# Attention, two gated layers, one core: per-lot waits before reloads, third lots behind the last store, and the last gate/value product inside the first output product

## What is computed

```python
# attention: B=4, HEADS=8, SEQ=576, HD=64; causal, window of 128 keys, ALiBi bias
scores = q @ k.T / 8 + slope[head] * -(i - j)        # only 0 <= i - j < 128
x = softmax(scores) @ v                              # -> 2304 tokens x 512
# layer 1: 512 -> 1024 -> 512
h = x @ w_in
solu = h * softmax(h)
x = (layernorm(solu) * g_ln) @ w_out
# layer 2: 512 -> 1536 -> 512
g = x @ w_gate
out = (g * sigmoid(g) * (x @ w_val)) @ w_out2
```

## Time and profile before

| | |
|---|---|
| median of 3 runs | 733.56 us (733.63, 731.66, 733.56) |
| the profiled execution | 733.14 us, of which span 731.4 us |
| granted TensorE clock, mean | 0.998 of full |
| TensorE busy | 715.9 us, 98% of the span |
| VectorE, ScalarE, GpSimd busy | 66%, 57%, 53% |
| the gate/value matmuls (L608) | 1512 matmuls, 505.6 us by their rows |
| the output matmuls (L767) | 756 matmuls, 254.6 us by their rows |

### The profile page before, as it was taken

How to read it: one execution, slowest core, us unless ns; L and a number is a source line. 1 busy time by engine, 2 the same in 40 slices (tenths; PEclk the granted TensorE clock), 3 DMA queues, 4 the chain that set the end, 5 groups by cost and what they waited for, 6 DMA issues and landing times.

```text
span 731.4 us, 13246 instructions
## 1 busy us (share of the span) xinstructions
PE 715.9 (98%) x4744; PEld 685.7 (94%) x4744; DVE 479.1 (66%) x850; ACT 415.5 (57%) x847; POOL 387.0 (53%) x398
## 2 busy tenths in 40 slices
PE   6999999999999999999999999999999999899998
PEld 5778999999999999999999999999999999899998
DVE  2887777777777777666885656555555699644551
ACT  5897777777777776474634433344443486345340
POOL 3567444445445445874938958759576918300000
PEclk9999999999999999999999999999999999999999
DMA  9723354433343323034234343324326753795722
GB/s 328 261 81 136 116 181 137 141 118 126 118 118 140 130 73 115 15 116 144 77 105 134 117 139 105 140 70 152 107 102 243 274 199 137 263 407 201 260 100 87
DMA packets 49340, 109.92 MB, mean 150 GB/s; under 512 B 3984, under 2 KB 30352, under 8 KB 49296
## 3 DMA queue, kind: packets, MB, share of 16 engines
q1 hardware_dynamic: 49296, 109.33, 43.3%
HBM read 75.11 MB, written 34.21 MB: 149 GB/s over the span
## 4 chain that ended last, share of the span: by engine, by line
PE 89%; DVE 3%; POOL 3%; DMA 2%; ACT 2%; issue 1%; SPq 0%; POOLq 0%; ACTq 0%; DVEq 0%
PE banks L608 35%; PE banks L594 14%; PE banks L567 14%; PE banks L767 14%; PE banks L553 4%; PE banks L539 2%; PE banks L580 2%; PE banks L530 2%; PE banks L531 2%; PE banks L517 2%; POOL st_sums L1498 2%; DMA lot_raw<-unit_scratch 1%; ACT xs_hi L783 1%; DMA unit_scratch<-st_sums 1%; DMA early<-in_first 1%
## 5 line engine op out<-in xcount | busy, mean ns | idle before, releaser
L608 PE MATMUL banks<-xs_hi,w_hi 128*128 128x384 f32 x504 | 168.8, 335 | 0.6 <-ACT g_sum L783 0.6
L608 PE MATMUL banks<-xs_hi,w_lo 128*128 128x384 f32 x504 | 168.4, 334 | 0.0
L608 PE MATMUL banks<-xs_lo,w_hi 128*128 128x384 f32 x504 | 168.4, 334 | 0.0
L608 PEld LDWEIGHTS banks<-xs_hi,w_hi 128*128 128x128 f32 x504 | 94.6, 188 | 1.6 <-ACT g_sum L783 1.1
L608 PEld LDWEIGHTS banks<-xs_lo,w_hi 128*128 128x128 f32 x504 | 94.6, 188 | 0.0
L608 PEld LDWEIGHTS banks<-xs_hi,w_lo 128*128 128x128 f32 x504 | 94.6, 188 | 0.0
L767 PE MATMUL banks<-lot_hi,wo_hi 128*128 128x384 f32 x252 | 85.1, 338 | 2.9 <-ACT out_a L783 2.2
L594 PE MATMUL banks<-lnt_hi,wout_hi 128*128 (+1 forms) x288 | 85.5, 297 | 0.0
L767 PE MATMUL banks<-lot_hi,wo_lo 128*128 128x384 f32 x252 | 84.8, 336 | 0.0
L767 PE MATMUL banks<-lot_lo,wo_hi 128*128 128x384 f32 x252 | 84.7, 336 | 0.0
L783 ACT ACTIVATE g_sum<-banks 128x384 f32<-128x384 f32 x84 | 41.1, 490 | 73.6 <-PE banks L608 56.6
(11 more groups left out here) (99 smaller groups left out, 1725.7 us busy)
## 6 DMA issues: line engine op xcount, KB each, us to landing
lot_raw<-unit_scratch SPq DMA_DIRECT2D x63, 384.0 KB, 4.9
qk_raw<-in_qk SPq DMA_DIRECT2D x28, 768.0 KB, 4.3
unit_scratch<-st_sums SPq DMA_DIRECT2D x18, 576.0 KB, 4.2
unit_scratch<-st_even SPq DMA_DIRECT2D x18, 384.0 KB, 2.5
unit_scratch<-st_odd SPq DMA_DIRECT2D x18, 384.0 KB, 3.2
w_raw<-in_wb SPq DMA_DIRECT2D x12, 512.0 KB, 4.5
v<-in_v SPq DMA_DIRECT2D x18, 256.0 KB, 2.6
x_scratch<-x_out SPq DMA_DIRECT2D x18, 256.0 KB, 2.6
```

Source lines behind the costliest of these rows:

```text
L608: last = mm(ps[n % 2], w_of[l][:, k * P:(k + 1) * P], x_of[r][:, k * HALF:(k + 1) * HALF], start=start and k == 0 and i == 0, stop=k == 1 ...
```

## The change

There are three edits.

1. `wait_stored` gets a lot number and waits only for the two chunk pairs of that lot, and SyncE's order is rewritten: the third lots of products 7 and 14 (lots 23 and 44) are loaded one step later than the first and second, and `store_pair(LAST - 2)` goes from step 1 to step 3, behind the loads of lots 21, 22, 24 and 25.
2. On TensorE, `product_3(LAST)` goes from behind the 18 matmuls of `out_product(0, 0)` to behind its first 9.
3. On ScalarE, at step `TILES`, the last two of six `xs_hi` copies of block 0 go behind `keep_p1(0)` and `keep_p7(0)`.

```diff
--- before.py
+++ after.py
@@ -283,11 +283,11 @@
                 if m >= 0:
                     eng.wait_ge(st_sent[m % 2], 48 * (m // 2 + 1))
 
-        def wait_stored(eng, j):
-
-            last = PAIRS.index(ORDER.index((C2 - 1, j)))
-            for b in range(2):
-                eng.wait_ge(st_sent[b], 48 * len(range(b, last + 1, 2)))
+        def wait_stored(eng, j, lot):
+
+            for c in (4 * lot + 1, 4 * lot + 3):
+                m = PAIRS.index(ORDER.index((c, j)))
+                eng.wait_ge(st_sent[m % 2], 48 * (m // 2 + 1))
 
         def op_ready(g):
 
@@ -441,8 +441,8 @@
                     sp.wait_ge(p3_ready, LAST + 1)
                 if g >= RING // LOTS:
                     sp.wait_ge(*op_ready(g - RING // LOTS))
-                if k % (7 * LOTS) == 0:
-                    wait_stored(sp, g // 7)
+                if g % 7 == 0:
+                    wait_stored(sp, g // 7, k % LOTS)
                 sp.dma_start(lot_raw[k % RING][:, :],
                              u_d[g // 7, OUT_OPS[g % 7][0], k % LOTS].rearrange("p h n -> p (h n)")
                              ).then_inc(lot_in[k % RING], 16)
@@ -479,11 +479,16 @@
                     sp.dma_start(out_d[rows, cols][:, :HALF], out_a[p][:, :]).then_inc(a_sent[p], 16)
 
             for g in range(OPS):
-                if g + RING // LOTS < OPS:
-                    for k in range(LOTS):
-                        load_lot(LOTS * (g + RING // LOTS) + k)
-                if g == 1:
-                    store_pair(LAST - 2)
+                ahead = g + RING // LOTS
+                if ahead < OPS:
+                    for k in range(LOTS - 1):
+                        load_lot(LOTS * ahead + k)
+                    if g == 3:
+                        store_pair(LAST - 2)
+                    if ahead % 7 == 1:
+                        load_lot(LOTS * ahead - 1)
+                    if ahead % 7:
+                        load_lot(LOTS * ahead + LOTS - 1)
                 if g == 5:
                     store_pair(LAST)
                 if g % 7 >= 4:
@@ -734,7 +739,7 @@
                     pe.wait_ge(solu_done, TILES)
                 period(n)
 
-            def out_product(g, p):
+            def out_product(g, p, chunks=range(CHUNKS2)):
 
                 j, o = g // 7, g % 7
                 n = LAST + 1 + 2 * j + p
@@ -758,7 +763,7 @@
                 if j == 0 and p == 0:
                     pe.wait_ge(wo_done, o + 1)
                 w_of = (wo_hi[o], wo_lo[OUT_OPS[o][1]])
-                for c in range(CHUNKS2):
+                for c in chunks:
                     lot = LOTS * g + c // 2
                     if p == 0 and c % 2 == 0:
                         pe.wait_ge(lot_done, lot + 1)
@@ -767,10 +772,12 @@
                         last = mm(ps[p], w_of[l][:, c, p * P:(p + 1) * P], lot_parts[lot % RING][r][:, cols],
                                   start=start and c == 0 and i == 0, stop=c == CHUNKS2 - 1 and i == 2,
                                   skip_group_check=not start)
-                last.then_inc(op_ready(g)[0], 1)
-
-            out_product(0, 0)
+                if chunks[-1] == CHUNKS2 - 1:
+                    last.then_inc(op_ready(g)[0], 1)
+
+            out_product(0, 0, range(0, 3))
             product_3(LAST)
+            out_product(0, 0, range(3, CHUNKS2))
             out_product(0, 1)
             for g in range(1, OPS):
                 for p in range(2):
@@ -913,7 +920,7 @@
                 if att:
                     exp_scores(t + 1, 0)
                 if is_at(t, TILES):
-                    for slot in X_ORDER[0][1:]:
+                    for slot in X_ORDER[0][1:5]:
                         xs_hi_part(0, slot)
                 if is_at(t, TILES + 1):
                     for slot in X_ORDER[1][:3]:
@@ -924,7 +931,9 @@
                 copy_x2(gx, f, spare)
                 if is_at(t, TILES):
                     keep_p1(0)
+                    xs_hi_part(0, X_ORDER[0][5])
                     keep_p7(0)
+                    xs_hi_part(0, X_ORDER[0][6])
                     keep_p16(0)
                     normalise(t - 1, 1 - odd)
                     for lot in (1, 2):
@@ -1057,7 +1066,7 @@
                 j = (n - LAST - 1) // 2
                 act_e.wait_ge(p3_ready, n + 1)
                 if j == 0:
-                    wait_stored(act_e, 0)
+                    wait_stored(act_e, 0, LOTS - 1)
                 else:
                     act_e.wait_ge(a_sent[n % 2], 16 * j)
                 copy(out_a[n % 2][:, :], ps_a[n % 2]).then_inc(out_a_done, 1)
```

## The result

The changed kernel takes 729.42 us (median of 6 runs, 729.32 to 729.77) against 733.60 us (median of 6 runs of the kernel before beside them, 731.66 to 735.76): a ratio of 0.9942, 95% interval 0.9924 to 0.9959, faster by 4.2 us. The forecast was 729.0.

What follows compares the result with a forecast made beforehand. TensorE, busy 98% of the span, was taken as the bound, with gains only where it stands still. Terms 3.94 - 0.15 + 0.3 = 4.1 us, from 733.14, gave 729.0 us; range 727.0 to 731.6 us.

Steps and rivals of the forecast that it cites:

- The break and its price (3.94 us): TensorE waits for ScalarE's `out_a` copy at product 7, between output blocks 0 and 1; removing this gains 3.94 us.
- Edit 1's path: Four lots load ahead of the store, so ScalarE copies `out_a` by 635.7, before TensorE asks at 636.99: 3.94 us gained.
- margin: At product 7, `out_a` would be ready 1.3 us before TensorE needs it, if lot 26 lands like the second load.
- Rival A: Lot 26 lands late, so the break at product 7 only shrinks: about 1.5 us given back, 730.5 us; chance 0.12.
- rival E: No effect: lot 26 lands at 638 as before and the break at product 7 stays whole, 733 us; chance 0.06.
- Edit 2 (0.15 lost): At the first output product, TensorE's wait moves to `val_b(LAST)` before `product_3(LAST)`; part 1 starts 0.15 us later.
- rival D: VectorE's 0.36 us break before 618.48 closes, shutting out GpSimd's first late sum: slower, 736.4 us; chance 0.06.
- Edit 3 (0.3 gained): In `period(0)`, `keep_p1(0)` comes earlier, but TensorE then waits 0.4 us for slot A22's `xs_lo`: 0.3 of 0.73 us gained.
- The sum: Over the whole kernel, the three edits' terms 3.94 - 0.15 + 0.3 give 4.1 us gained.
- B: The clock falls after 0.98 us idle at the new `val_b` wait at 592.9: 1.6 us lost, 730.6 us; chance 0.05.
- C: GpSimd's last pair sums (period LAST) lengthen by 11.5 us; TensorE's product 10 waits 2.2 us: 731.2 us; chance 0.05.

Runs made afterwards that it cites:

- the one with slot A22 first: The changed kernel with VectorE's `lot_lo` of lot 2 behind `val_b(LAST)` and slot A22's `xs_lo` ahead of tile 17's statistics: 729.05 us, ratio 0.9945.

## Why the prediction was right, point by point

- **The break and its price (3.94 us).** Right, from the rows of the kernel before: edit 1 alone gains 3.92 in the output stage. The split into 2.37 idle and 1.57 clock and restart was nearly right; filling the gap gives back 1.31, and 1.57 less TensorE's restart (0.11) and the 0.13 us by which product 7 came later there is 1.33. What made the forecast meet the median as well is in part luck: it went by one execution, in which the clock fell, and so it did in 30 of 46. Had the median fallen among the other 16, it would have been 2.3 us that were gained and not 4.1.
- **Edit 1's path.** Right in each place: lots 21, 22, 24 and 25 loaded ahead of the store, `out_a` copied by 635.83 with the sums late (working: 635.7), margin over 1 us. Rival A (lot 26 late) is what the run with lots 24 and 25 behind the store shows on purpose; in the changed kernel it didn't happen, and neither did rival E: lots 23 to 26 were copied from 631.13 to 634.18.
- **Edit 2 (0.15 lost).** On TensorE's own path right: 133.00 against 132.86 is 0.14. But the sentence that calls edit 2 a mere move of a wait missed its side effect: alone, it gains 2.64 us by letting GpSimd in. The prediction had the mechanism in rival D, with the wrong sign and a wrong condition. It took VectorE's break of 0.36 us before 618.48 for the only door. But the sum ended at 618.53 and needs 1.02 us, so it was in before the break began; the door was the `g_sum` at 617.56, which reads a bank and comes whether there is a break behind it or not. The door that opened after the change was a pause of 0.08 us at 615.4, and it opened because TensorE came later against VectorE.
- **Edit 3 (0.3 gained).** Somewhat too large. The product on slot A22 started 3.96 us after the first gate/value matmul and starts 3.68 after it now: 0.28. Two slips cancel in that: the old wait had a restart behind it (0.11) that the working left out, and the wait on `xs_lo` is longer than worked out, 0.56 us from start to start where it was 0.42 (the idle row reads 0.39). The restart behind the new wait then takes 0.11, and at the transposes of tile 17 7.08 us became 6.91: 0.17. By the first output matmul 0.06 of it is left in the changed kernel's trace; a wait on `xs_lo` of TensorE's weight load at 366.7 reads 0.42 us there where it read 0.31. All the traces together say 0.2: five with edit 3 (without the one with slot A22 first) took 277.56 to 277.67 us from the first gate/value to the first output matmul, seven without it 277.72 to 277.88.
- **The sum.** 4.1 forecast; 3.78 in the output stage and 0.06 before it are 3.84, and the medians differ by 4.2. The difference of 0.3 us is small beside what the opening (312.35 to 314.08) and the clock add from execution to execution.
- **Rivals B and C.** The clock held at 1.00 over the 0.80 us of idle time at 594. GpSimd's last sums (period LAST) took 1.02, 1.62, 1.73 and 1.54 us beside VectorE's `lot_lo`: GpSimd was first, as said, and was not shut out.

What the right number hides is that the break had three separate cures (the order of the loads, earlier sums, the place of the `out_a` copy), and the change applied two of them. The gain would have been the same without edit 2.

## What to carry to other kernels

When a long chain ends in a short copy that frees a bank, look first at what that copy stands behind on its own engine: moving one `out_a` copy gained all that the reordered loads did. A GpSimd instruction much longer than its neighbours of the same shape may be waiting, as this one was; here a pause in VectorE's work, even one of 0.08 us, or a deliberate one where VectorE had slack, shortened it. A change of a tenth of a us elsewhere can open or close such a pause, so compare these rows before crediting an edit. Take changes apart even when the sum comes out right.

## What the runs showed of the hardware

- A GpSimd addition of 128x384 from SBUF took 1.02 us when VectorE's instruction beside it read a bank or VectorE was idle, and 3.50, 5.57, 9.72 or 12.49 us when it was issued into an unbroken row of VectorE subtractions with both operands in SBUF. It ended 0.96 to 0.98 us after the start of that row's first pause (0.06 to 0.08 us sufficed) or first instruction that reads a bank. Once in, it took turns with VectorE without further pauses, and three VectorE subtractions took 5.10 us instead of 2.69.
- In the profiled executions TensorE's clock stood at the 2.4 GHz level after idle times of 0.69, 0.80, 0.83 and 0.85 us in the output stage and fell to the 1.2 GHz level in those of 2.20 and 2.31 us; filled with matmuls, the same 2.4 us left it up. In 16 of 46 executions of the kernel before the mean granted clock was 1.000, so the fall is not certain there either.
- A wait that was added on VectorE, 1.50 us long, made the output stage 3.9 us shorter (132.87 us instead of 136.78).
